# Half of each tile's score matmuls behind the transposes of the last tile's probabilities

## The reference

```python
# q, k, v: (4, 8, 576, 64)
k_p = k.reshape(B, H, S // 8, 8, D).mean(axis=3)      # 72 keys for each head
v_p = v.reshape(B, H, S // 8, 8, D).mean(axis=3)
scores = (1 / sqrt(D)) * q @ k_p.T
attn = exp(scores - max(scores)); attn = attn / (sum(attn) + 1e-9)
x = attn @ v_p                      # as 2304 rows of 512
xn = x / sqrt(mean(x * x) + 1e-6) * rms_g
x = (silu(xn @ w_gate) * (xn @ w_val)) @ w_out        # 512 -> 1536 -> 512
out = silu(x @ w_in) @ w_out2                         # 512 -> 2048 -> 512
```

## Time and profile before

| | us |
|---|---|
| median of 3 runs (lowest, highest) | 862.01 (861.58, 862.6) |
| the profiled execution | 862.45 |
| its span | 860.7 |
| TensorE busy | 850.8 (99%) |
| VectorE busy | 551.4 (64%) |
| GpSimd busy | 421.2 (49%) |
| ScalarE busy | 360.0 (42%) |
| TensorE's granted clock | 0.999 of full speed |

### The profile page before, as it was taken

The page is one execution under the profiler, slowest core; times in us unless marked ns, Lnnn a source line. Parts: engine busy times, 40 slices in busy tenths (PEclk is TensorE's granted clock), DMA queues, the critical chain, the costliest instruction groups (busy, mean ns, idle before and its releaser), DMA issues.

```text
span 860.7 us, 13899 instructions
## 1 busy us (share of the span) xinstructions
PE 850.8 (99%) x5292; PEld 830.6 (96%) x5292; DVE 551.4 (64%) x835; ACT 360.0 (42%) x640; POOL 421.2 (49%) x415
## 2 busy tenths in 40 slices
PE   7999999999999999999999999999999999999998
PEld 6999999999999999999899899999999999999998
DVE  6689757875545579955664345569634798335873
ACT  3689845543221325545553221324333444134521
POOL 6898999883427480577763044380161700004300
PEclk9999999999999999999999999999999999999999
DMA  9971578778869987565779489997789748687762
GB/s 255 269 218 42 221 262 318 271 303 311 326 223 407 407 329 266 200 260 223 278 292 370 160 294 362 356 400 262 268 287 361 252 189 286 250 330 253 253 238 102
DMA packets 94801, 235.78 MB, mean 274 GB/s; under 512 B 23056, under 2 KB 69136, under 8 KB 83216
## 3 DMA queue, kind: packets, MB, share of 16 engines
q1 hardware_dynamic: 94736, 234.90, 75.9%
HBM read 164.10 MB, written 70.78 MB: 273 GB/s over the span
## 4 chain that ended last, share of the span: by engine, by line
PE 96%; DMA 2%; POOL 1%; DVE 0%; SPq 0%; issue 0%; DVEq 0%; POOLq 0%
PE ps L2001 17%; PE ps L2003 17%; PE ps L2002 17%; PE ps L2139 5%; PE ps L2138 5%; PE ps L2137 5%; PE ps L2099 3%; PE ps L2097 3%; PE ps L2098 3%; PE ps L1931 3%; PE ps L2068 3%; PE ps L2069 3%; PE ps L2067 3%; PE ps L2044 2%; PE ps L2043 2%; PE ps L2042 2%
## 5 line engine op out<-in xcount | busy, mean ns | idle before, releaser
L2001 PE MATMUL ps<-xh,wr 128*128 128x384 f32 x840 | 282.9, 337 | 0.3
L2003 PE MATMUL ps<-xh,wr 128*128 128x384 f32 x840 | 281.3, 335 | 0.0
L2002 PE MATMUL ps<-xl,wr 128*128 128x384 f32 x840 | 281.0, 335 | 0.0
L2001 PEld LDWEIGHTS ps<-xh,wr 128*128 128x128 f32 x840 | 157.6, 188 | 4.4 <-DVE qt L1570 1.5
L2002 PEld LDWEIGHTS ps<-xl,wr 128*128 128x128 f32 x840 | 157.8, 188 | 0.3
L2003 PEld LDWEIGHTS ps<-xh,wr 128*128 128x128 f32 x840 | 157.7, 188 | 0.0
L2138 PE MATMUL ps<-ew,efh 128*128 128x256 f32 x336 | 95.1, 283 | 0.0
L2139 PE MATMUL ps<-ew,efl 128*128 128x256 f32 x336 | 95.1, 283 | 0.0
L2137 PE MATMUL ps<-ew,efh 128*128 128x256 f32 x336 | 95.1, 283 | 0.0
L1589 DVE TENSOR_TENSOR qt<-ps,qt 128x384 f32<-128x384 f32 x84 | 46.4, 556 | 49.8 <-PE ps L2003 49.7
L950 POOL TENSOR_TENSOR eh<-eh 128x768 f32<-128x768 f32 x8 | 17.2, 2168 | 122.8 <-DVE efl L1666 122.8
(11 more groups left out here) (198 smaller groups left out, 1767.1 us busy)
## 6 DMA issues: line engine op xcount, KB each, us to landing
wr<-ring_home SPq DMA_DIRECT2D x40, 1792.0 KB, 9.7
ring_home<-wr SPq DMA_DIRECT2D x20, 1792.0 KB, 8.0
ew<-ending_home SPq DMA_DIRECT2D x8, 2048.0 KB, 8.5
out_home<-wo SPq DMA_DIRECT2D x14, 1024.0 KB, 9.4
fw<-fold_home SPq DMA_DIRECT2D x8, 1536.0 KB, 7.8
ew<-out_home SPq DMA_DIRECT2D x24, 512.0 KB, 7.2
fw<-out_home SPq DMA_DIRECT2D x18, 512.0 KB, 6.6
ending_home<-eb SPq DMA_DIRECT2D x16, 512.0 KB, 10.8
```

Source lines behind the costliest of these rows:

```text
L2001: pe.matmul(out_ps, w_hi, x_hi, start=first and c == 0, stop=False, skip_group_check=True)
L2002: pe.matmul(out_ps, w_hi, x_lo, start=False, stop=False, skip_group_check=True)
L2003: ins = pe.matmul(out_ps, w_lo, x_hi, start=False, stop=c == 1, skip_group_check=True)
```

## The change

TensorE's scores of a tile become two steps. The first half (column chunks 0 and 1, the first bank) stays where the scores were, with all their waits. The second half (chunks 2 and 3) comes behind the transposes of the last tile's probabilities and ahead of the queries of the next tile; `s_sc` is raised there. In step 0 no transposes stand between the halves. The other engines' programs are the same: they do not know the step `scores2` and pass over it. In a split tile each half has eight matmuls on 64 columns.

```diff
         if 0 <= s - 1 < NT:
             order.append(("prT", s - 1))
+
+        if s < NT:
+            order.append(("scores2", s))
         if s + 1 < NT:
             order.append(("q", s + 1))
...
-            def scores(n):
-                pe.wait_ge(s_qTc, n + 1)
-                pe.wait_ge(s_kTc, parts(n)[-1][0] + 1)
-                if n == 0:
-                    pe.wait_ge(s_khalf, 1)
-                else:
-                    pe.wait_ge(s_shift, n)
+            def scores(n, half):
+                if half == 0:
+                    pe.wait_ge(s_qTc, n + 1)
+                    pe.wait_ge(s_kTc, parts(n)[-1][0] + 1)
+                    if n == 0:
+                        pe.wait_ge(s_khalf, 1)
+                    else:
+                        pe.wait_ge(s_shift, n)
                 for b, r0, m in parts(n):
-                    for c in range(KC):
+                    for c in range(2 * half, 2 * half + 2):
                         last = pe.matmul(sc_ps[r0:r0 + m, c // 2, (c % 2) * 2 * SP:(c % 2 + 1) * 2 * SP],
                                          qT[:, c, r0:r0 + m], kT[b % 2][:, c * 2 * SP:(c + 1) * 2 * SP],
                                          start=True, stop=True)
-                last.then_inc(s_sc, 1)
+                if half == 1:
+                    last.then_inc(s_sc, 1)
...
                 elif what == "scores":
-                    scores(n)
+                    scores(n, 0)
+                elif what == "scores2":
+                    scores(n, 1)
```

## The result

The changed kernel takes 863.50 us (median of 13 runs, 862.58 to 865.84) against 862.08 (13 runs) for the kernel before: a ratio of 1.0020, 95% interval 1.0012 to 1.0027, so 1.0 to 2.3 us slower. The profiled execution took 863.5 us, its span 861.8.

What follows compares the result with a forecast made beforehand. TensorE, busy in 99% of the span, was taken as the bound, with VectorE's chain pacing from tile 9. Lateness summed to 0.74 - 0.10 = 0.64, so +0.6 us on the median 862.01: forecast 862.6, range 860.9 to 864.3.

Steps and rivals of the forecast that it cites:

- rival B: VectorE's subtraction ahead of tile 17's maximum waits up to 1.1 us for GpSimd: 1.7 slower, 863.7; chance 0.20.
- The waits and the copy: Usual tiles: transposes and copy come 0.52 us earlier, the values' 0.16 wait goes, up to 11 x 0.16 = 1.8 us.
- a longer hole at the key transposes near 65: TensorE's early 0.44 us and later won waits end as idle time there, growing from 0.46 to about 1 us.
- Up to tile 9: Lateness summed from 24.91: tile 9's scores 0.44 us early, its maximum +0.11 late.
- The split term: Tiles 4 and 13: one more pair of switches between narrow and full matmuls, +0.29 us each, twice 0.58.
- that wait: Tile 5, one tile behind split tile 4: the value product's wait for ScalarE's copy goes, -0.16 us.
- The chain from tile 9: VectorE's rows from tile 9's maximum on have no holes, so its +0.11 us is passed on.
- Tiles 14 to 17: Row maxima there come late by +0.32, +0.59, +0.74 and +0.74 us, with VectorE idle until the scores.
- The step of the late semaphore: Scores' semaphore comes 0.55 us later, so a maximum starts 1.80 behind its scores; tile 14 to 15 forecast at 0.27.
- The forecast's +0.64 at the end of the stage: TensorE leaves the attention stage late by tile 17's 0.74 less 0.10, 0.64 us, with no later hole to absorb it.
- The collision: VectorE's subtraction near 85.7 and GpSimd's 2.06 us operation lock each other out; VectorE waits up to 1.1 us; chance 0.20.
- 0.2 us apart in my working: Expected starts ahead of tile 17's maximum: GpSimd's operation at 85.5, VectorE's subtraction at 85.7; the first to start decides.

Runs made afterwards that it cites:

- the repetition: The unchanged changed kernel measured and profiled a second time, beside the kernel before: 863.56 us against 861.91, ratio 1.0017.
- the two runs: The changed kernel (863.50 us), and the changed kernel with tiles 4 and 13 left whole ahead of the transposes (863.20 us).
- the run without the collision: Changed kernel with GpSimd's last two low parts of unit 0's weights moved ahead of tile 13's mean square: 862.70 us, ratio 1.0011 to the kernel before.
- the turns: Kernel before with the two row halves of split tiles 4 and 13 taking turns chunk by chunk: 862.33 us, ratio 1.0007.

## Why the prediction was right or wrong

The time lies in the range and on the side to which the forecast leaned. But what came is rival B, given 0.20, and not the forecast, given 0.58: it cost 0.6 + 1.1 = 1.7 in the text, 1.4 measured.

**The waits and the copy: right**, in the usual tile, 3.96 for 3.99. What TensorE wins by it was to end as a longer hole at the key transposes near 65. That hole is 0.46 us as before; it ends at 60.41 instead, where TensorE waits for VectorE's division.

**Up to tile 9: the sum met by luck.** Tile 9's maximum was forecast at +0.11 and is at +0.13 in the first profile (50.81, with 0.49 put back). But in the three others with the same order up to there it is 0.23 to 0.27 early (51.33 in the repetition, -0.26). Two errors and an accident meet in the one number. The split term has the wrong sign: I took two switches for +0.29 and the split tile became 0.29 shorter. The switches do cost, 0.21 by the two runs; what I didn't see is that the edit also changes the order of the narrow matmuls, from four chunks and four chunks to two and two, and that this gives 0.50. Of this gain a part is lost again one tile later, where ScalarE's queue waits for GpSimd's root, in before too (0.91 us at 32.23, 1.15 in the first profile of after at 32.13, 0.75 in its repetition), and the value product for ScalarE's copy behind it. I had listed that wait as gone. The accident is the hole of 0.36 at GpSimd in the first profile: with it the value product at 34.11 finds TensorE idle for 0.47 us and comes 0.13 late against the keys (34.47 in before); in the repetition (34.62) TensorE is not idle there, and it is 0.27 early.

**The chain from tile 9: right in what it carries, too simple in what holds it.** I took VectorE's queue for the bound. It is held at 52 us by GpSimd's sums, and moves with their start. In the run with the new order in tiles 1 to 8 alone a maximum 0.39 early got nothing, as GpSimd's start was not earlier; in the repetition of after, GpSimd was 0.26 early and the chain with it.

**Tiles 14 to 17: right in kind, large in size.** Forecast +0.32, +0.59, +0.74 for tiles 14, 15 and 16, found +0.15, +0.52, +0.52, in the repetition -0.24, +0.14, +0.13, with the idle time on VectorE that I named. The step of the late semaphore, tile 14 to 15, was forecast at 0.27 and is 0.37 or 0.38. The forecast's +0.64 at the end of the stage is near the run without the collision (+0.47 in the stage, +0.79 in time), but by other terms: there the maximum of tile 17 is at +0.14, where the forecast had +0.74, and 0.3 us come behind it.

**The collision: place and price right, chance wrong.** I named this subtraction and up to 1.1 us; it is 1.13 (2.08 against 0.95), and 1.07 of it arrives at the next maximum. The step that failed is "0.2 us apart in my working", from which I gave it 0.20. By that working GpSimd comes first (85.5 against 85.7), so it spoke for the rival and not for the forecast. And the two are far closer. In before VectorE is 0.04 us ahead; GpSimd is 0.01 or 0.02 ahead in after, in its repetition, in the new order up to tile 13, in that up to tile 8 and in the turns; and where the split tiles are whole they are level, and VectorE kept its own time. They are close because both hang on tile 15: VectorE through its own queue (in after also through tile 16's scores, 0.23 us of idle time ahead of 83.02), GpSimd through the exponential, the squares and the mean square. In before the subtraction follows tile 15's maximum by 6.33 us (78.71 to 85.04), in the run with tiles 1 to 8 by 6.41 (77.98 to 84.39), because the operation between (80.78 and 80.04) took 1.26 in the one and 1.34 in the other. So an edit that moves a few hundredths of a microsecond can turn it over. The Trainium skill (SBUF — State Buffer, SBUF: two separate sides) states that whichever of the two starts first holds the port pair for its whole instruction; the eight profiles in which one of the two has a lead at this place agree, down to a lead of 0.01 us.

What stays open is how often VectorE comes second in each kernel. The profiles show it once each, or twice for the changed kernel; where tiles 4 and 13 are whole, VectorE kept its time in the profile, and the kernel is as slow in its times as those in which it came second.

## What to carry to other kernels

An engine that is never idle may still be paced by another one that it meets at a shared resource; time won ahead of the meeting is passed on only as far as the other engine has won it too. Before an edit is credited or blamed for a microsecond, look for two operations that start within a few hundredths of each other and swap durations between the profiles, and repeat the comparison with that meeting taken away. Take a second profile of the same kernel before a difference of some tenths is explained: here 0.4 us of the first was its own. And when a loop is cut in two, check what the cut does to the order inside it.

## What the runs showed of the hardware

Narrow matmuls on the two column halves of the array gain from standing close together in the queue: 16 of 128 x 64 took 1.68 us to the next full one in two groups of eight, 1.13 taking turns chunk by chunk, and 1.18 (26.95 to 28.13) in four groups of four. A pair of switches to narrow and back cost 0.21 us.

The operations of 0.95 us (VectorE) and 1.27 us (GpSimd) took 2.07 to 2.09 and 2.05 to 2.09 us when they came second by 0.05 us or less. When it was 0.10 or 0.13 us behind, the second took 2.00 or 1.96. In each of these profiles the one that came first kept its own time, and the second ended 2.09 to 2.11 us behind the first one's start.
